# Keeping the split first-layer weights of a seven-product channel MLP in DRAM between token tiles

## The reference

```python
gamma = 1 - 2 ** (-5 - arange(H)); state = 0
for t in range(S):
    state = gamma * state + outer(k[t], v[t])      # per batch and head
    y[t] = q[t] @ state / sqrt(D)
x = heads of y side by side                        # 2 x 768 x 512
u = x + ((x^T @ U) @ V)^T                          # U: 768 x 32, V: 32 x 768
x2 = u + relu(u @ w_ch1) @ w_ch2                   # 512 -> 2048 -> 512
h = relu(x2 @ w_in); a, b = halves of h            # 512 -> 1024
bn = (b - mean(b)) / sqrt(var(b) + 1e-6)
out = (a * (w_spatial @ bn + b_spatial)) @ w_out   # w_spatial: 768 x 768
```

## Time and profile before

| what | value |
|---|---|
| median of three runs | 486.72 us |
| the profiled execution's own time | 485.45 us |
| its span, first to last instruction | 483.7 us |
| mean granted clock of TensorE | 0.996 of full |
| PE / DVE / ACT / POOL busy | 97% / 69% / 48% / 27% |
| matmuls, weight loads | 3176 each |
| DMA moved | 50.31 MB, mean 104 GB/s |

### The profile page before, as it was taken

How to read it: one execution, slowest core, us unless ns; L and a number is a source line. 1 busy time by engine, 2 the same in 40 slices (tenths; PEclk the granted TensorE clock), 3 DMA queues, 4 the chain that set the end, 5 groups by cost and what they waited for, 6 DMA issues and landing times.

```text
span 483.7 us, 8542 instructions
## 1 busy us (share of the span) xinstructions
PE 468.4 (97%) x3176; PEld 418.4 (87%) x3176; DVE 332.5 (69%) x643; ACT 232.8 (48%) x540; POOL 129.0 (27%) x110
## 2 busy tenths in 40 slices
PE   8999986999998999999998999999999999999997
PEld 4788785989897988888897888888998889999997
DVE  4888878769999988556779978555772775521530
ACT  2765754546658555434557555433552752221212
POOL 2285952223443312222243212221232040000000
PEclk9999998999999999999999999999999999999999
DMA  8999502083222222022222222112214300011003
GB/s 288 409 306 312 197 1 87 18 303 118 87 88 89 87 88 88 5 84 87 88 87 89 88 87 88 39 50 87 88 45 186 130 0 1 1 66 65 1 0 131
DMA packets 19929, 50.31 MB, mean 104 GB/s; under 512 B 1456, under 2 KB 3120, under 8 KB 18608
## 3 DMA queue, kind: packets, MB, share of 16 engines
q1 hardware_dynamic: 19472, 49.24, 29.3%
q10 hardware_dynamic: 416, 0.53, 0.3%
HBM read 46.61 MB, written 3.15 MB: 103 GB/s over the span
## 4 chain that ended last, share of the span: by engine, by line
PE 87%; DVE 7%; DMA 2%; ACT 2%; issue 1%; SPq 0%; DVEq 0%; ACTq 0%
PE bank L1231 10%; PE bank L1142 8%; PE bank L1144 8%; PE bank L1145 8%; PE bank L1126 7%; PE bank L1128 7%; PE bank L1129 7%; PE bank L1246 7%; PE bank L1184 2%; PE bank L1182 2%; PE bank L1183 2%; PE bank L995 2%; DVE w1cl L791 2%; PE bank L1040 2%; PE bank L1034 2%; DVE bl L797 1%
## 5 line engine op out<-in xcount | busy, mean ns | idle before, releaser
L432 POOL TENSOR_TENSOR w2l<-w2raw,w2h 128x512 fp32r<-128x512 f32 x48 | 67.9, 1418 | 207.6 <-ACT w2h L547 207.6
L1126 PE MATMUL bank<-bh,w1ch 128*128 128x256 f32 x336 | 95.6, 284 | 7.7 <-DVE hl L816 6.5
L1129 PE MATMUL bank<-bh,w1cl 128*128 128x256 f32 x336 | 95.0, 283 | 0.0
L1128 PE MATMUL bank<-bl,w1ch 128*128 128x256 f32 x336 | 94.9, 282 | 0.0
L1126 PEld LDWEIGHTS bank<-bh,w1ch 128*128 128x128 f32 x336 | 63.9, 190 | 16.0 <-DVE w1cl L791 5.8
L1142 PE MATMUL bank<-hh,w2h 128*128 128x512 f32 x192 | 76.2, 397 | 0.0
L1144 PE MATMUL bank<-hl,w2h 128*128 128x512 f32 x192 | 76.1, 397 | 0.0
L1145 PE MATMUL bank<-hh,w2l 128*128 128x512 f32 x192 | 75.0, 391 | 0.0
L1128 PEld LDWEIGHTS bank<-bl,w1ch 128*128 128x128 f32 x336 | 63.9, 190 | 5.5
L808 DVE TENSOR_TENSOR c<-bank,p 128x256 f32<-128x256 f32 x72 | 30.3, 421 | 50.3 <-PE bank L1129 41.2
L1129 PEld LDWEIGHTS bank<-bh,w1cl 128*128 128x128 f32 x336 | 63.7, 190 | 0.0
(11 more groups left out here) (119 smaller groups left out, 893.2 us busy)
## 6 DMA issues: line engine op xcount, KB each, us to landing
w1raw<-w SPq DMA_DIRECT2D x24, 512.0 KB, 5.1
w2raw<-w SPq DMA_DIRECT2D x24, 512.0 KB, 4.1
att<-attn SPq DMA_DIRECT2D x7, 1152.0 KB, 8.3
att<-attn SPq DMA_DIRECT2D x10, 384.0 KB, 5.3
out_T<-stage SPq DMA_DIRECT2D x7, 384.0 KB, 2.3
wsp_raw<-w_sp SPq DMA_DIRECT2D x1, 2304.0 KB, 8.3
winraw<-w_in SPq DMA_DIRECT2D x1, 2048.0 KB, 9.3
tab<-decay SPq DMA_DIRECT2D x7, 258.0 KB, 4.7
```

The costliest lines, as they stand in the source:

```text
L432: nc.gpsimd.tensor_tensor(w2l[h][:, :], w2raw[n % 2][:, h, :], raw(w2h[h])[:, :], ALU.subtract).then_inc(w2_lo, 1)
L1126: mm(o, w1ch[k][:, q, s], bh[:, q, c, :], start=(opens and c == 0), stop=False, skip_group_check=True)
L1128: mm(o, w1ch[k][:, q, s], bl[:, q, c, :], start=False, stop=False, skip_group_check=True)
L1129: m = mm(o, w1cl[k][:, q, s], bh[:, q, c, :], start=False, stop=(c == 1), skip_group_check=True)
```

## The change

The two tiles `w1ch` and `w1cl` of a buffer become one tile `w1c` (rounded part at index 0, rest at 1), and a DRAM tensor `w1_split` holds all eight blocks in split form. In slots 0 to 7 nothing of the splitting changes, except that SP stores each finished block to DRAM (1.835 MB per store), and that ACT waits for the store of block `n - 2` before it writes block `n` over it. From slot 8 on, `weight_sums`, `round_w1` and `rest_w1` do nothing; SP loads the split block (1.835 MB) in place of the raw one, as soon as product 6 of slot `n - 2` is done, and PE waits for that load at product 0. Slots 8 and 9 wait for the last stores first.

Further: the first w2 block is loaded ahead of the second w1 block and split in pair 4 (both halves); the first two operands of w1 block 1 are rounded in pair 5; of the token operands of tile 0, numbers 2 and 3 are rounded ahead of `p_round` in pair 6 and number 4 behind it. On VectorE the three `rest_hid` come ahead of the remaining `rest_b` at the end of a tile, and in slot 0 ahead of `u_add` and `rest_w1(1, 6)`, with `rest_w1(1, 5)` between the second and the third.

The diff with unchanged lines cut:

```diff
--- before.py
+++ after.py
@@ -94,11 +94,10 @@
         bl, o = at("bl", o, [P, NQ, 2, HT], f32r)
-        w1ch, w1cl, w1raw, w2raw, w2h, w2l, hh, hl = ([None, None] for _ in range(8))
+        w1c, w1raw, w2raw, w2h, w2l, hh, hl = ([None, None] for _ in range(7))
         o = W1C_AT
         for k in range(2):
-            w1ch[k], o = at(f"w1ch{k}", o, [P, NQ, 2 * P], f32r)
-            w1cl[k], o = at(f"w1cl{k}", o, [P, NQ, 2 * P], f32r)
+            w1c[k], o = at(f"w1c{k}", o, [P, 2, NQ, 2 * P], f32r)
         o = W1R_AT
@@ -154,6 +153,8 @@
 
+        w1_split = nc.dram_tensor("w1_split", [NP, P, 2, NQ, 2 * P], f32, kind="Internal").ap()
+
         bank = [ctx.enter_context(nc.psum_tensor(f"bank{i}", [P, 512], f32)) for i in range(8)]
@@ -175,6 +176,8 @@
         w1_loaded = [sem(f"w1_loaded{k}") for k in range(2)]
+        split_stored = [sem(f"split_stored{k}") for k in range(2)]
+        split_loaded = [sem(f"split_loaded{k}") for k in range(2)]
         w2_loaded = [sem(f"w2_loaded{k}") for k in range(2)]
@@ -345,15 +348,23 @@
                 load_v(i + 2, k)
-                if i == 0:
-                    load_w1(0)
-                elif i == 2:
-                    load_w1(1)
-                elif i == 3 or i == 4:
-                    load_w2(i - 3)
+                if i == 0 or i == 3:
+                    load_w1(i // 3)
+                elif i == 2 or i == 4:
+                    load_w2(i // 2 - 1)
             for n in range(2, NN):
-                sp.wait_ge(w1_lo, NQ * (n - 1))
-                load_w1(n)
+                if n < NP + 2:
+                    sp.wait_ge(w1_lo, NQ * (n - 1))
+                    if n < NP:
+                        load_w1(n)
+                    sp.dma_start(w1_split[n - 2, :, :, :, :], raw(w1c[n % 2])[:, :, :, :]
+                                 ).then_inc(split_stored[n % 2], 16)
+                if n >= NP:
+                    if n < NP + 2:
+                        sp.wait_ge(split_stored[n % 2], 16 * (NP // 2))
+                    sp.wait_ge(pr_done, NQ * (n - 1))
+                    sp.dma_start(raw(w1c[n % 2])[:, :, :, :], w1_split[n % NP, :, :, :, :]
+                                 ).then_inc(split_loaded[n % 2], 16)
                 sp.wait_ge(w2_lo, 2 * (n - 1))
@@ -407,7 +418,7 @@
                     pool.wait_ge(w1_hi, q + 1)
-                    nc.gpsimd.tensor_tensor(w1cl[0][:, q, :], w_operand(0, q), raw(w1ch[0])[:, q, :],
+                    nc.gpsimd.tensor_tensor(w1c[0][:, 1, q, :], w_operand(0, q), raw(w1c[0])[:, 0, q, :],
                                             ALU.subtract).then_inc(w1_lo, 1)
@@ -451,6 +462,8 @@
                     first_weight_rest(range(4, NQ))
+                    rest_w2(0, 0)
+                    rest_w2(0, 1)
                 elif i == 5:
@@ -461,9 +474,10 @@
                     n = t * NP + j
+                    if n > 1:
+                        rest_w2(n - 1, 1)
                     if n:
-                        rest_w2(n - 1, 1)
-                    rest_w2(n, 0)
+                        rest_w2(n, 0)
                     if t and j == 2:
@@ -517,7 +531,7 @@
             def round_w1(n, qs):
-                if n >= NN:
+                if n >= NP:
                     return
@@ -527,7 +541,8 @@
                         act.wait_ge(pr_done, NQ * (n - 2) + q + 1)
-                    nc.scalar.activation(w1ch[k][:, q, :], w_operand(k, q), ACT.Copy).then_inc(w1_hi, 1)
+                        act.wait_ge(split_stored[k], 16 * (n // 2))
+                    nc.scalar.activation(w1c[k][:, 0, q, :], w_operand(k, q), ACT.Copy).then_inc(w1_hi, 1)
 
@@ -604,7 +619,17 @@
                     round_w1(0, range(2, NQ))
+                elif i == 4:
+                    round_w2(0, 0)
+                elif i == 5:
+                    round_w1(1, range(0, 2))
+                elif i == 6:
+                    round_b(0, range(2, 4))
                 p_round(i - 1)
+                if i == 4:
+                    round_w2(0, 1)
+                elif i == 6:
+                    round_b(0, range(4, 5))
                 if i == 1:
@@ -615,7 +640,7 @@
                 elif i == 6:
-                    round_b(0, range(2, NQ))
+                    round_b(0, range(5, NQ))
             xn_copy(NI - 1, 0)
@@ -625,9 +650,10 @@
                         xn_copy(NI - 1, 1)
-                    else:
+                    elif n > 1:
                         round_w2(n - 1, 1)
-                    round_w1(n + 1, range(0, 2))
+                    if n:
+                        round_w1(n + 1, range(0, 2))
                     if final:
@@ -649,7 +675,8 @@
                     relu_hid(n, 1)
-                    round_w2(n, 0)
+                    if n:
+                        round_w2(n, 0)
                     relu_hid(n, 2)
@@ -783,12 +810,12 @@
             def rest_w1(n, qs):
-                if n >= NN:
+                if n >= NP:
                     return
...
                     dve.wait_ge(w1_hi, NQ * n + q + 1)
-                    nc.vector.tensor_tensor(w1cl[k][:, q, :], w_operand(k, q), raw(w1ch[k])[:, q, :],
+                    nc.vector.tensor_tensor(w1c[k][:, 1, q, :], w_operand(k, q), raw(w1c[k])[:, 0, q, :],
                                             ALU.subtract).then_inc(w1_lo, 1)
@@ -909,22 +936,21 @@
                     rest_w1(n + 1, range(4, 5))
+                    sum_c(n, 2)
+                    if n:
+                        rest_w1(n + 1, range(5, 6))
+                    rest_hid(n, 0)
+                    if n:
+                        rest_w1(n + 1, range(6, 7))
+                    rest_hid(n, 1)
+                    if n == 0:
+                        rest_w1(n + 1, range(5, 6))
+                    rest_hid(n, 2)
+                    if n == 0:
+                        rest_w1(n + 1, range(6, 7))
+                        u_add(NI - 1)
                     if final:
-                        rest_b(t + 1, range(2, 4))
-                    sum_c(n, 2)
-                    if n == 0:
-                        u_add(NI - 1)
-                    rest_w1(n + 1, range(5, 6))
-                    rest_hid(n, 0)
-                    if final:
-                        rest_b(t + 1, range(4, 5))
-                    rest_hid(n, 1)
-                    rest_w1(n + 1, range(6, 7))
-                    if final:
-                        rest_b(t + 1, range(5, 6))
-                    rest_hid(n, 2)
-                    if final:
-                        rest_b(t + 1, range(6, 7))
+                        rest_b(t + 1, range(2, NQ))
                     if t and j == 1:
@@ -1099,7 +1125,10 @@
                 o = (x, z, x, y, x, y, x)[q]
-                pe.wait_ge(w1_lo, NQ * n + q + 1)
+                if n < NP:
+                    pe.wait_ge(w1_lo, NQ * n + q + 1)
+                elif q == 0:
+                    pe.wait_ge(split_loaded[k], 16 * ((n - NP) // 2 + 1))
                 if n % NP == 0:
@@ -1123,10 +1152,10 @@
                     s = slice(c * P, (c + 1) * P)
-                    mm(o, w1ch[k][:, q, s], bh[:, q, c, :], start=(opens and c == 0), stop=False,
+                    mm(o, w1c[k][:, 0, q, s], bh[:, q, c, :], start=(opens and c == 0), stop=False,
                        skip_group_check=True)
-                    mm(o, w1ch[k][:, q, s], bl[:, q, c, :], start=False, stop=False, skip_group_check=True)
-                    m = mm(o, w1cl[k][:, q, s], bh[:, q, c, :], start=False, stop=(c == 1), skip_group_check=True)
+                    mm(o, w1c[k][:, 0, q, s], bl[:, q, c, :], start=False, stop=False, skip_group_check=True)
+                    m = mm(o, w1c[k][:, 1, q, s], bh[:, q, c, :], start=False, stop=(c == 1), skip_group_check=True)
                 m.then_inc(pr_done, 1)
```

## The result

The changed kernel is slower: 489.42 us in the median of 11 runs (488.61 to 489.95), against 487.65 for the kernel before in its 11 runs beside it. The ratio is 1.0041, with a 95% interval of 1.0027 to 1.0055, so 2.0 us more (1.3 to 2.7). The forecast was 484.8 and faster. The profiled execution of the changed kernel took 489.61 us, its span 487.7, which is 4.0 more than the span before. That execution of before took 485.45 us, 2.2 less than the median of the 11, so the difference of the two profiles is larger than the ratio says; which stretch of before varies from run to run by a microsecond or two stays open.

What follows compares the result with a forecast made beforehand. TensorE, busy 97% of the span, was taken as the bound, so only its waits and low clock could be won. Terms -1.3 - 4.3 - 1.7 + 5.8 = -1.5, with small waits -1.9, gave 484.8 us, range 478.2 to 488.

Steps and rivals of the forecast that it cites:

- Term 1: Pair 6, before the scores at 61.15: token-block roundings moved off ACT's path let the scores start earlier, -1.3 us.
- Pairs 4 and 5: GpSimd and ACT work moved into pairs 4 and 5 fills idle gaps there and changes nothing, 0 us.
- Term 2: Slot 0 to slot 1: `hl` ready sooner, so 2.9 us less stall and no 1.4 us of low clock, -4.3 us.
- Term 3: The two later tile starts: `hl` waits of 2 x 1.45 us vanish, 0.6 us each lost on `sum_c`, -1.7 us.
- The 0.3 us of slot 7: Small waits in slot 7, 0.3 us, expected to go and counted in addition to the terms.
- Term 4: Slot 3: ACT waits for block 2's store behind `winraw`; 4.4 us stall plus 1.4 us of low clock, +5.8 us.
- The other stores and loads: 0: Stores of blocks 4 and 5 and loads of slots 8 and 9 land before they are needed, 0 us.
- rival C: Transfers at 305 GB/s, 1.7 us more each; slots 3, 5, 6 and 9 stall longer: slower, 491.8 us, chance 0.13.
- Rival B: Slot 3: the store of block 2 is hidden, terms 1 to 3 stay whole, -7.7 us: 479.0 us, chance 0.22.
- Rival D: Gains cancel: GpSimd's contention eats term 1 or 3, ACT bounds slot 0's chain: 486 to 487.5 us, chance 0.10.
- The removed work: Relief of VectorE and GpSimd, which have idle time of their own, is worth nothing by itself.

Runs made afterwards that it cites:

- reordering-only kernel: The changed kernel without stores or loads of split blocks, every weight block split in its slot as before: 480.94 us, ratio 0.9881 to the kernel before.
- kernel with the DRAM part alone: The kernel before plus only the DRAM tensor, its stores, loads and waits, all other work in the old order: 496.43 us, ratio 1.0195.
- the best version: The changed kernel with stores and raw loads issued one step earlier and three bl rests moved behind a tile's first sum_c: 476.98 us, ratio 0.9797.
- the same order without a DRAM part: The changed kernel without split stores or loads, and with three bl rests moved behind a tile's first sum_c: 478.78 us, ratio 0.9836.
- the early stores: The changed kernel with each store and raw load issued one w2raw load earlier in SP's list: 478.51 us, ratio 0.9833 to the kernel before.

## Why the prediction was wrong, by its own steps

**Term 1** (-1.3) held: the wait before the scores of pair 7 fell from 1.45 to 0.12 us; the gain shows as 0.8 because this execution was already 0.5 late in pair 3.

**Pairs 4 and 5** (0) held: there is no stall there.

**Term 2** (-4.3) held to a tenth. PE resumed at 76.16, 1.94 us into slot 1 (forecast 1.96), at full clock. The reordering-only kernel repeats it.

**Term 3** (-1.7) held in place and gave -1.3: slot 16 is 0.6 us shorter and slot 8, without the wait for load 9, 0.7. Each start still takes 11.45 us for 10.53, 0.9 lost on `sum_c` (0.7 of it wait) where 0.6 was said. The 0.3 us of slot 7, counted beside the terms, held. Most of this is the removed work and not the new order: with the old order the wait for `hl` is down to 0.20 us too, and slot 16 is shorter still.

**Term 4** (+5.8) was right in place and mechanism and 1.5 us too small: slot 3 lost 7.3. ACT's wait on store 2 stalled product 4 by 5.51 us (4.4 forecast), with 0.2 for the refill and 1.6 at the low clock behind it (1.4). The store landed 19.9 us after slot 2's start, forecast 18.8. By its packets it began at 14.1 (13.4 forecast; `winraw` and the raw load ahead were slower than in the profile before), lasted 5.4 us (4.3) and landed 0.35 behind its last packet (1.0). The last of these is luck: a landing priced too long hid half of what the transfer was priced too short.

**"The other stores and loads: 0"** is the step that failed. They cost 0.7 and 1.05 us in slots 5 and 6 and 1.7 ahead of slot 9 (the wait of 1.56 with the first matmul's refill), 3.5 us in all. The forecast difference -1.9, with term 4's 1.5 and these 3.5, gives +3.1; the 0.4 missing from term 3 and the 0.5 of the late first pairs make it the +4.0 of the profiles, and the ratio says +2.0. The 29 MB of added traffic in that paragraph are a slip, too: eight stores and sixteen loads of 1.835 MB, less sixteen raw blocks, are the 35.6 MB measured. I had priced a store by the best slice of the trace, 442 GB/s, and set the next transfer right behind its last byte. What queued transfers really did is in slices of the changed kernel (busy us of PE, PEld, DVE, ACT and POOL, then clock, DMA share, GB/s). The first two lie in the raw pair with store 4 behind it, the next two in store 4; the last three are load 8, store 7 and load 9:

```profile
121.00:122.00 1.00, 1.00 (x9) 0.91 (x8) 0.49 (x2) 0.73 (x2) 0.00 (x0) 1.00 0.68 127
122.00:123.00 1.00, 1.00 (x9) 0.96 (x8) 1.00 (x4) 0.71 (x2) 0.00 (x0) 1.00 0.80 127
125.00:126.00 1.00, 1.00 (x10) 1.00 (x9) 1.00 (x2) 0.11 (x1) 1.00 (x1) 1.00 1.00 430
128.00:129.00 1.00, 1.00 (x8) 0.87 (x8) 0.96 (x2) 0.00 (x0) 0.36 (x1) 1.00 0.28 115
149.00:157.00 8.00, 8.00 (x53) 7.22 (x52) 5.37 (x8) 5.74 (x14) 2.12 (x3) 1.00 0.83 258
157.00:164.00 7.00, 6.33 (x40) 5.42 (x39) 5.46 (x8) 2.71 (x7) 2.63 (x2) 1.00 0.75 309
165.00:171.00 6.00, 4.95 (x28) 3.97 (x26) 4.32 (x9) 1.84 (x4) 1.30 (x1) 1.00 0.88 329
```

In its middle a store does run at the forecast rate, 430 GB/s. The rest of the time lies around it. The raw pair ahead took 5.45 us of packets (119.23 to 124.68), with a hole of two slices at 127 GB/s, where 3.6 was assumed; the store's own packets last from 123.64 to 128.94, 5.3 us where 4.3 was assumed, and it lands 0.4 behind. So store 4 landed at 129.30, 4.3 us into slot 5, where +2.5 was forecast and +3.7 was the limit that the text itself gives. From first packet to last the eight stores take 5.1 to 6.8 us and the sixteen loads 4.9 to 7.5, so both are above the 4.3, and neither is the quicker as a whole. They differ inside: a store's packets take 0.54 us each throughout, 128 of them on 16 DMA engines, and eight in a row are the 4.3; what comes on top lies at its two ends, where not all engines are on it. The packets of all loads but one take 0.61 to 0.66 in the mean. Load 9 averages 329 GB/s over its middle and takes 6.95 us from issue to landing. In the chain of four transfers load 9 landed at 171.47, 13.1 us into slot 8 (158.34), where +8.6 was forecast: 4.5 us late, 1.1 per link.

The warning stood in the trace of before. `winraw`'s 2.1 MB needed 6.4 us of packets there, 329 GB/s over the whole transfer, while its best slice shows 442. By the whole transfer each link would have been 5.6 us and not 4.3, and stores 4 and 5 would have passed their limit. Put through rival C's own steps, as an estimate, 1.3 us more per transfer are 1.3 in slot 3, 0.1 each in slots 5 and 6 and 4 x 1.3 - 2.5 = 2.7 before slot 9: 4.2 us more, 489.0.

**Rival B** is out: nothing of store 2 was hidden, ACT waited 7.66 us. **Rival C** was right in kind, at about two thirds of its price per link (1.1 us for 1.7), and with another cause: it is not the packets of a store that are slow, but the start and the tail of each transfer, the holes in the raw pair and the packets of the loads. It named all three places, slots 5, 6 and 9. Its turning point, 0.9 us more per transfer, was passed, and with it the sign. The Trainium skill's limit of about 358 GB/s for a core (DMA: Bandwidth & Descriptors, Specifications), half of what it gives for two cores together, did not hold as a ceiling for this one core: stores ran at 430 in their middle, and one load kept 372 over its whole 4.93 us. That the other loads stay at 245 to 325 over theirs has a cause that no run here shows.

**Rival D** did not occur in its own form: no gain was eaten whole. GpSimd has its part in what term 3 fell short, though: at slot 16 two of the five `bl` lie beside its `w2l` and take 1.29 and 1.78 us, the other three 0.68.

**The removed work** was rightly priced at nothing wherever nobody waited for it. Of VectorE's 85 us and ACT's 35 us hardly more than those at slot 7 and the tile starts count: 0.3 us and 1.1 in slots 7 and 16 of the kernel with the DRAM part alone, against before, and 1.5 in all between the best version and the same order without a DRAM part.

What stays open: why a pair of raw loads is slower with a third transfer queued behind it (no run takes that apart), what makes the packets of loads take longer than those of stores, what decides how long the lower clock lasts behind a stall, and why the two profiles differ by 4.05 us where the timed runs differ by 2.0.

## What to carry to other kernels

Price a chain of queued transfers by the time that a whole transfer takes from issue to landing, start and tail included, and not by the best slice of a long one; then compare each landing with the instruction that waits for it, to the microsecond. A wait for a landing in an engine's list holds all that stands behind it, so issue the transfer at the semaphore that makes its data ready, ahead of waits that belong to other work: here that one reordering of SP's list turned 0.4% slower into 1.7% faster, and with one sum moved ahead of three rests into 2.0%. Work taken from engines that have idle time wins only where it stood in front of something that the busiest engine waits for; read in the timeline what stands there.

## What the runs showed of the hardware that was not expected

- A pair of 512 KB loads with a 1.8 MB store queued behind it took 5.45 us of packets; in the kernel before, with nothing behind them, such pairs took 3.7 to 4.6, most of them under 4.1.
- The 1.8 MB transfers differ by direction in their packets of 14,336 B, 0.54 us each in stores and 0.61 to 0.66 in the mean of 15 of the 16 loads, and hardly in whole: 5.1 to 6.8 us from first packet to last for stores, 4.9 to 7.5 for loads. From issue to landing the median of the 16 loads is 7.4 us, that of the 8 stores, most of them behind other transfers, 10.7. The page after, section 6 (KB each, median us to landing):

```profile
w1c<-w_split SPq DMA_DIRECT2D x16, 1792.0 KB, 7.4
w_split<-w1c SPq DMA_DIRECT2D x8, 1792.0 KB, 10.7
```

- Traffic of 86 MB in place of 50, a mean of 180 GB/s, did not slow TensorE: with the early stores its slots last the same 10.53 us as in the kernel before.
- Beside GpSimd a `bl` rest that takes 0.68 us alone took 1.78, more than the 0.87 in the mean suggested, and it is such an instruction that stands ahead of `sum_c` at a tile start. GpSimd's `w2l` ran from 269.00 to 270.46 there; the `bl`, begun at 269.24, ended at 271.02, 0.56 us behind it, as if it had not started until then.
- The price of the lower clock behind a stall is not fixed. Stalls of 4.0 to 5.5 us were followed by 1.3 to 2.8 us of loss at the lower clock (the same 4.0 us by 1.3 in one kernel and 2.6 in another), one of 2.23 us by 1.5, one of 2.32 us by none.
